# Three reorderings of small steps in a fused attention and expert kernel: first second-weight split, open groups, low parts at the border

## The chip, the cores and the metric

The kernel runs on one core of a Trainium2 chip. The metric is the device time of one execution in microseconds, as the median of several runs. The engines are TensorE (PE; its weight loads are PEld), VectorE (DVE), ScalarE (ACT), GpSimd (POOL) and SyncE (SP), which here issues all DMAs.

## What is computed

All inputs and outputs are float32. With 2 batches of 576 tokens, 8 heads of 64, a model width of 512:

```python
# 1. attention: pooled (means over 4 tokens) plus local (|i - j| < 4), per head
x = repeat(softmax(q_d @ k_d.T / 8) @ v_d, 4) + softmax(where(|i-j|<4, q @ k.T / 8, -1e9)) @ v
# 2. first network, 512 -> 2048 -> 512
h = x @ w_in
y = where(h > 0, h, exp(min(h, 0)) - 1) @ w_out
# 3. four experts, 512 -> 1024 -> 512, all on all 1152 tokens, weighted by normalised probabilities
p = domain_probs / (domain_probs.sum(-1) + 1e-9)
out = sum(p[:, e] * (relu(y @ w1[e]) @ w2[e]) for e in range(4))
```

## The kernel before, in words

**High and low parts.** Each float32 matrix product is done as three matmuls on rounded values (fp32r): high by high, high by low, low by high. So each operand is split. ScalarE copies the raw tile to a rounded high part (`wa_hi`, `wb_hi`, `x_hi`, `h_hi`), and GpSimd (weights, and layer 3's inputs) or VectorE (`x_lo`, `h_lo`) subtracts it from the raw tile for the low part. The helper `product` issues the three matmuls of each chunk (lines 437 to 439), `product2` the same for the experts (514 to 518). A weight tile is 128 x 4 x 512: four chunks of 128 x 512, for which `wa_` holds a block of the first weights of a network and `wb_` one of the second weights. There is one raw, one high and one low buffer of each. SyncE loads the next block into `wa_raw` or `wb_raw` when all four low parts of the block before are done (`next_wa`, `next_wb`, lines 286 and 291).

**Stages.** (1) Attention of the first batch, four head pairs one after the other, with nothing else on TensorE. (2) The first network for batch 0, as four blocks of 512 hidden units; each has 16 groups of 12 matmuls of 288 columns. Groups 0 to 7 make hidden tiles (and wait for `wa_lo`), groups 8 to 15 apply the second weights (and wait for `wb_lo`). Attention of one head pair of the second batch is spread between the groups (`mixed_block1`). The first of the four blocks is written out by itself, the others are a loop. (3) The same network for batch 1, again four blocks, the first by itself. (4) The experts: eight halves (expert and half of its hidden units). Each half has two steps, `step2(j, b)`, for the two sets of tokens, and then `down2`, which multiplies the hidden tiles by the second weights, four token tiles first and five later, each 12 matmuls of 512 columns. `step2` needs sums of weight quarters beside the weights: GpSimd makes these with four additions and subtractions (`add_w2`, lines 1201 to 1206), in `wa_raw` and a small area, and ScalarE and GpSimd split them together with the weights (`split_w2`, `split_wa2`).

**Order.** Each engine runs its own list, written out by hand, and waits on semaphores that count what others finished. Nothing is reordered at run time.

**Group and PSUM banks in layer 2.** Groups go through four PSUM banks. Group g of the first eight is followed by ScalarE's relu and exp (`elu_parts`, lines 710 and 713), VectorE's maximum (941), ScalarE's `h_hi` (719) and VectorE's `h_lo` (947), and only then is the bank free: group g + 4 waits for `h_lo` of group g (`bank_free1`). ScalarE's list for group g is: `elu_parts(g)`, then what stands in `between` for that group (parts of attention), then `elu_hi(g - 1)`, then for g = 0, 1, 2 one, one and two of the four `wb_hi` copies (`split_wb`, line 702).

**Open groups (`up_first`).** In the first block of either batch the last input tile `x` (chunk 3) comes late. So TensorE takes the first `OPEN` = 4 groups side by side: the matmuls of chunks 0, 1 and 2 for all four groups, then those of chunk 3 for all four. Between chunk 2 and chunk 3 of batch 0 stand the input transposes of the next head pair (line 355).

**Before the first mixed block** ScalarE ends stage 1 with `split_x(3, 0, 3)`, the last input tile, and then waits for the transposes (`copy_qT`).

**The border from layer 2 to 3.** `step2(0, 0)` and `step2(0, 1)` run, then `down2` of half 0, four tiles, then `step2(1, 0)`. GpSimd's list there is: `split_y(1)` (low parts of the second batch's inputs), `add_w2(1)`, `split_wb(8)` (the four `wb_lo` of half 0's second weights), `split_wa2(1)`. The last three are the first pass of a loop over the halves. ScalarE makes the four `wb_hi` of half 0 in `step2(0, 1)`, the last of them after two `h_hi`, and then splits the next half's weights and sums (`next_weights2`). VectorE copies the gate column of the expert (`gate_now`, line 1022) before the first use in `down2` (line 1026).

Of the kernel before, what the change touches and what calls it, by code (L numbers as in the profile page):

```python
# [45 lines left out]
FC = FB // 128  # L46
BLOCKS1 = D_FF // FB
# [4 lines left out]
GROUPS1 = T1 * FC + T1 * KC  # L52
# [9 lines left out]
HALVES = EXPERTS * HALVES2  # L62
# [13 lines left out]
DOWN2_BANKS = (7, 6)  # L76
BANK_A, BANK_B, BANK_C = (0, 3), (1, 4), (2, 5)
OUT_SPLIT = QT * SPANS[1][1]
OPEN = 4

# [13 lines left out]
def program(nc, q, k, v, w_in, w_out, probs, w1, w2, out):  # L96
# [12 lines left out]
    with ExitStack() as ctx:  # L109
# [3 lines left out]
        def sem(name):  # L113
            return ctx.enter_context(nc.semaphore(name))
# [98 lines left out]
        s_raw_ready, s_hi_ready, s_lo_ready = sem("s_raw_ready"), sem("s_hi_ready"), sem("s_lo_ready")  # L213
# [124 lines left out]
        def _(pe):  # L338
# [5 lines left out]
            def turn_in(u, mode):  # L344

                if mode == MIXED:
                    pe.wait_ge(out_free, 2 * u + OUT_CREDIT)
                for n, src in enumerate((q_in[held(u)], k_in[held(u)])):
                    pe.wait_ge((q_loaded, k_loaded)[n][held(u)], 32 * loads(u))
                    if n == 1 and mode == ALONE and u >= 2:  # L350

                        pe.wait_ge(attnT_p_copied, 2 * (u - 1))
                        pe.wait_ge(attnT_copied, 3 * (u - 1) - 1)
                    for c in range(NLT):
                        last = nc.tensor.transpose(psum[:, IN_BANKS[mode][n] + c // 3, LT * (c % 3):LT * (c % 3 + 1)],  # L355
                                                   src[:, c, :], ident[0:LT, 0:LT])
                    last.then_inc(in_turned, 1)
# [116 lines left out]
            def up_first(w, b):  # L474

                for k in range(KC):
                    pe.wait_ge(wa_lo_ready, KC * w + k + 1)
                    if b == 0 and k == KC - 1:
                        turn_in(HALF_PAIRS, MIXED)
                    pe.wait_ge(x_lo_ready, KC * b + k + 1)  # L480
                    for g in range(OPEN):
                        if k == 0:
                            bank_free1(w, g)
                        cols, t = slice(128 * g, 128 * (g + 1)), slice(b * SEQ, b * SEQ + N1)
                        bank = psum[:, MOE_BANKS[g], 0:N1]
                        nc.tensor.matmul(bank, wa_hi[:, k, cols], x_hi[:, k, t], start=(k == 0), stop=False)
                        nc.tensor.matmul(bank, wa_hi[:, k, cols], x_lo[:, k, t], start=False, stop=False)
                        last = nc.tensor.matmul(bank, wa_lo[:, k, cols], x_hi[:, k, t], start=False, stop=(k == KC - 1))
                        if k == KC - 1:
                            last.then_inc(group_done, 1)  # L490

            def mixed_block1(i, u):

                if isinstance(i, int):
                    up_first(i, 0)
                for g in range(GROUPS1):
                    if not isinstance(i, int) or g >= OPEN:
                        group1(i, 0, g)
                    if g == 0 and not isinstance(i, int):
                        turn_in(u, MIXED)  # L500
                    elif g == 3:
                        score(u, 0, MIXED)
                        score(u, 1, MIXED)
                    elif g == 5:
                        score(u, 2, MIXED)
                    elif g in (7, 9, 11):
                        turn_attn(u, (g - 7) // 2, MIXED)
                    elif g == 13:
                        mix(u, MIXED)
# [128 lines left out]
                mixed_block1(i, i + HALF_PAIRS)  # L638

            up_first(BLOCKS1, 1)  # L640
            for g in range(OPEN, GROUPS1):
                group1(BLOCKS1, 1, g)
            with pe.Fori(BLOCKS1 + 1, 2 * BLOCKS1) as w:
                for g in range(GROUPS1):
# [9 lines left out]
        def _(act):  # L654
            def copy_qT(u, mode):
                first = IN_BANKS[mode][0]
                act.wait_ge(in_turned, 2 * u + 1)

                nc.scalar.activation(qT[:].rearrange("p (a n) -> p a n", a=2), psum[:, first:first + 2, 0:HALF], ACT.Copy,
                                     scale=HD ** -0.5).then_inc(qT_copied, 1)  # L660
# [29 lines left out]
            def split_x(u, b, i):  # L690
                act.wait_ge(out_free, OUT_CREDIT + 2 * u + 2)
                nc.scalar.copy(x_hi[:, i, b * SEQ:(b + 1) * SEQ], x_sum[:]).then_inc(x_hi_ready, 1)
# [23 lines left out]
            def elu_hi(w, b, g):  # L716
                t0 = b * SEQ + N1 * (g // FC)
                act.wait_ge(elu_ready, UP1 * w + g + 1)
                nc.scalar.copy(h_hi[:, g % FC, t0:t0 + N1], psum[:, MOE_BANKS[g % 4], 0:N1]).then_inc(h_hi_ready, 1)

            def group1(w, b, g, between=(), next_wa=True):
                if g < UP1:
                    elu_parts(w, g)
                for step, *where in between:
                    step(*where)
                if 1 <= g <= UP1:
                    elu_hi(w, b, g - 1)
                if g < FC - 1:
                    split_wb(w, g)
                if g == FC - 2:  # L730
                    split_wb(w, FC - 1)
                if next_wa and g >= UP1 and g < UP1 + KC:
                    split_wa(w + 1, g - UP1, groups_before1(w) + UP1)
# [98 lines left out]
            for u in range(HALF_PAIRS):  # L832
                for j in range(3):
                    if j > 0:
                        copy_attnT(u, j, ALONE)
                    if u + 1 < HALF_PAIRS:
                        exponentiate(u + 1, j, ALONE)
                if u + 2 < HALF_PAIRS:
                    copy_qT(u + 2, ALONE)
                copy_pooled(u, ALONE)  # L840
                if u == 0:
                    first_wa(0)
                if u + 1 < HALF_PAIRS:
                    first_wa(u + 1)
                split_x(u, 0, u)
            copy_qT(HALF_PAIRS, MIXED)

            def mixed_block1(i, u):

                between = {  # L850
                    0: [] if isinstance(i, int) else [(copy_qT, u, MIXED)],
                    3: [(exponentiate, u, 0, MIXED)],
                    4: [(exponentiate, u, 1, MIXED)],
                    6: [(exponentiate, u, 2, MIXED)],
                    10: [(copy_attnT, u, 1, MIXED)],
                    12: [(copy_attnT, u, 2, MIXED)],
                    14: [(copy_pooled, u, MIXED)],
                    15: [(split_x, u, 1, i)],
                }
                for g in range(GROUPS1):  # L860
                    group1(i, 0, g, between.get(g, ()))

            mixed_block1(0, HALF_PAIRS)
            with act.Fori(1, BLOCKS1) as i:
# [269 lines left out]
        def _(pool):  # L1134
# [31 lines left out]
            def split_wb(w):  # L1166
                for c in range(FC):
                    split_w(w, c, wb_raw, wb_hi, wb_lo, wb_hi_ready, wb_lo_ready)
# [29 lines left out]
            def add_w2(j):  # L1198

                pool.wait_ge(wa_loaded, 16 * (2 * BLOCKS1 + j + 1))  # L1200
                nc.gpsimd.tensor_tensor(s_raw[:, S1], wa_quad(1, 0), wa_quad(1, 1), ALU.add).then_inc(s_raw_ready, 1)
                pool.wait_ge(s_raw_ready, 4 * j + 1)
                nc.gpsimd.tensor_tensor(s_raw[:, S2], s_raw[:, S1], wa_quad(0, 0), ALU.subtract).then_inc(s_raw_ready, 1)
                nc.gpsimd.tensor_tensor(wa_quad(1, 0), wa_quad(0, 0), wa_quad(1, 0), ALU.subtract).then_inc(s_raw_ready, 1)
                pool.wait_ge(s_raw_ready, 4 * j + 3)
                nc.gpsimd.tensor_tensor(s_raw[:, S4], wa_quad(0, 1), s_raw[:, S2], ALU.subtract).then_inc(s_raw_ready, 1)
# [6 lines left out]
            def split_wa2(j):  # L1213

                w = 2 * BLOCKS1 + j
                split_w(w, 0, wa_raw, wa_hi, wa_lo, wa_hi_ready, wa_lo_ready)
                split_w(w, 1, wa_raw, wa_hi, wa_lo, wa_hi_ready, wa_lo_ready)
                split_s(j, S2)
                split_w(w, 2, wa_raw, wa_hi, wa_lo, wa_hi_ready, wa_lo_ready)
                split_w(w, 3, wa_raw, wa_hi, wa_lo, wa_hi_ready, wa_lo_ready)  # L1220
                split_s(j, S1)
                split_s(j, S4)
# [54 lines left out]
            add_w2(0)  # L1277
            split_wa2(0)
            split_y(1)
            with pool.Fori(0, HALVES - 1) as j:  # L1280
                pool.wait_ge(s_lo_ready, 3 * j + 3)
                add_w2(j + 1)
                split_wb(j + 2 * BLOCKS1)
                split_wa2(j + 1)
# [22 lines left out]
```

## Time and profile before

| | us |
|---|---|
| median of 3 runs | 676.61 (676.55 to 676.63) |
| the profiled execution | 676.82 |
| its span, first to last instruction | 674.8 |
| TensorE busy in it | 655.0 (97%) |
| mean granted TensorE clock | 0.994 of full speed |

The profile is one execution of the program, taken by the hardware profiler. All times in it count from the start of the span; the execution takes 2.0 us beside the span. L12 is line 12 of the kernel. A row of the timeline reads: start, duration, engine, line, operation, output and inputs, shape, count and, in brackets, how long the engine sat idle before it and what ended that. A granted clock of 1.00 is 2.4 GHz, of 0.50 is 1.2 GHz.

### The profile page before, as it was taken

How to read it: one execution, taken by the hardware profiler on the slowest of the kernel's cores; microseconds unless marked ns; L12 is line 12 of the kernel's file. 1: busy time of each engine (PE TensorE's matmuls, PEld its weight loads, DVE VectorE, ACT ScalarE, POOL GpSimd, SP SyncE). 2: the span in 40 equal slices, each digit the busy share in tenths (PEclk: the TensorE clock that was granted, in tenths of full speed). 3: DMA queues.
4: the chain of work that ended last, by engine and by line, in shares of the span. 5: the costliest groups of instructions: out<-in, count | busy, mean ns of one | idle time of the engine just before them, and what ended most of it. 6: DMA issues, size and time to landing. Idle time of an engine off the chain costs nothing.

```text
span 674.8 us, 12939 instructions
## 1 busy us (share of the span) xinstructions
PE 655.0 (97%) x4750; PEld 601.8 (89%) x4756; DVE 325.1 (48%) x714; ACT 277.6 (41%) x759; POOL 304.4 (45%) x266
## 2 busy tenths in 40 slices
PE   7988999999989999998999999999999999999998
PEld 4767999999989999997889989998998899899886
DVE  4784454545444433465345436534544454365342
ACT  3756565656555653745115214214133152152110
POOL 3584343535349832879605606325337147061110
PEclk9999999999989999999999999999999999999999
DMA  9944070605102123110201201103003012010012
GB/s 173 240 80 157 5 196 6 192 3 159 62 28 99 63 72 115 63 63 34 92 1 63 64 0 62 62 0 124 0 0 124 0 49 75 1 62 1 1 48 93
DMA packets 51488, 46.11 MB, mean 68 GB/s; under 512 B 31616, under 2 KB 33920, under 8 KB 51456
## 3 DMA queue, kind: packets, MB, share of 16 engines
q1 hardware_dynamic: 51456, 45.67, 23.0%
q8 instruction: 21, 0.34, 0.2%
q14 instruction: 11, 0.09, 0.0%
HBM read 43.30 MB, written 2.36 MB: 68 GB/s over the span
## 4 chain that ended last, share of the span: by engine, by line
PE 85%; ACT 6%; DVE 4%; POOL 3%; issue 1%; DMA 1%; SPq 0%; POOLq 0%; ACTq 0%; DVEq 0%
PE psum L437 19%; PE psum L439 18%; PE psum L438 18%; PE psum L516 8%; PE psum L518 8%; PE psum L514 8%; ACT attn L670 2%; ACT attn_p L670 1%; DVE neg_max L899 1%; POOL x_lo L1190 1%; PE psum L429 1%; PE psum L355 1%; PE psum L408 1%; POOL wb_lo L1160 1%; PE psum L374 1%
## 5 line engine op out<-in xcount | busy, mean ns | idle before, releaser
L1160 POOL TENSOR_TENSOR wb_lo<-wb_raw,wb_hi 128x512 fp32r<-128x512 f32 x64 | 82.0, 1294 | 215.3 <-ACT wb_hi L702 215.3
L1026 DVE SCALAR_TENSOR_TENSOR o_acc<-psum,gate_now,o_acc 128x512 f32<-128x512 f32 x72 | 54.1, 751 | 129.8 <-PE psum L439 129.4
L437 PE MATMUL psum<-wb_hi,h_hi 128*128 128x512 f32 x288 | 112.9, 392 | 2.6 <-POOL wb_lo L1160 2.6
L439 PE MATMUL psum<-wb_hi,h_lo 128*128 128x512 f32 x288 | 112.9, 392 | 0.0
L438 PE MATMUL psum<-wb_lo,h_hi 128*128 128x512 f32 x288 | 112.8, 392 | 0.0
L759 ACT ACTIVATE h_hi<-psum 128x320 fp32r<-128x320 f32 (+1 forms) x128 | 52.4, 411 | 87.8 <-DVE psum L998 40.4
L1160 POOL TENSOR_TENSOR wa_lo<-wa_raw,wa_hi 128x512 fp32r<-128x512 f32 x60 | 76.0, 1295 | 23.6 <-ACT wa_hi L746 14.1
L765 ACT COPY sums<-psum 128x256 f32<-128x256 f32 (+1 forms) x32 | 12.8, 399 | 163.3 <-PE psum L518 163.3
L437 PE MATMUL psum<-h_hi,wb_hi 128*128 128x288 f32 x256 | 76.8, 300 | 0.0
L439 PE MATMUL psum<-h_hi,wb_lo 128*128 128x288 f32 x256 | 75.4, 294 | 0.0
L438 PE MATMUL psum<-h_lo,wb_hi 128*128 128x288 f32 x256 | 75.4, 294 | 0.0
L437 PE MATMUL psum<-x_hi,wa_hi 128*128 128x288 f32 x224 | 68.3, 305 | 4.9 <-DVE h_lo L947 4.5
L437 PEld LDWEIGHTS psum<-wb_hi,h_hi 128*128 128x128 f32 x288 | 54.4, 189 | 13.9 <-issue 2.9
L438 PE MATMUL psum<-x_lo,wa_hi 128*128 128x288 f32 x224 | 66.7, 298 | 0.0
L439 PE MATMUL psum<-x_hi,wa_lo 128*128 128x288 f32 x224 | 66.7, 298 | 0.0
L439 PEld LDWEIGHTS psum<-wb_hi,h_lo 128*128 128x128 f32 x288 | 54.4, 189 | 11.4
L438 PEld LDWEIGHTS psum<-wb_lo,h_hi 128*128 128x128 f32 x288 | 54.5, 189 | 11.1
L980 DVE SCALAR_TENSOR_TENSOR h_lo<-psum,h_hi 128x320 fp32r<-128x320 f32 (+1 forms) x128 | 54.9, 450 | 17.0 <-ACT h_hi L759 17.0
L518 PE MATMUL psum<-x_hi,wa_lo 128*128 128x256 f32 (+1 forms) x192 | 56.8, 296 | 0.0
L516 PE MATMUL psum<-x_lo,wa_hi 128*128 128x256 f32 (+1 forms) x192 | 56.7, 295 | 0.0
L514 PE MATMUL psum<-x_hi,wa_hi 128*128 128x256 f32 (+1 forms) x192 | 56.6, 295 | 0.0
L941 DVE SCALAR_TENSOR_TENSOR psum<-sums,psum 128x288 f32<-128x288 f32 x64 | 29.6, 462 | 48.0 <-ACT sums L713 47.8
(146 smaller groups left out, 1548.3 us busy)
## 6 DMA issues: line engine op xcount, KB each, us to landing
wa_raw<-in_moe_w_in SPq DMA_DIRECT2D x8, 1024.0 KB, 5.5
wb_raw<-in_moe_w_out SPq DMA_DIRECT2D x8, 1024.0 KB, 5.0
wa_raw<-in_moe_w SPq DMA_DIRECT2D x8, 1024.0 KB, 4.9
wb_raw<-in_moe_w SPq DMA_DIRECT2D x8, 1024.0 KB, 5.0
out<-o_acc SPq DMA_DIRECT2D x9, 256.0 KB, 2.0
q_in<-in_q SPq DMA_DIRECT2D x10, 144.0 KB, 3.5
k_in<-in_k SPq DMA_DIRECT2D x10, 144.0 KB, 4.0
v_in<-in_v SPq DMA_DIRECT2D x5, 288.0 KB
```

Source lines behind the costliest of these rows:

```text
L437: nc.tensor.matmul(bank_cols, w_hi(n), x_hi_(n), start=(n == 0), stop=False)
L438: nc.tensor.matmul(bank_cols, w_hi(n), x_lo_(n), start=False, stop=False)
L439: last = nc.tensor.matmul(bank_cols, w_lo(n), x_hi_(n), start=False, stop=(n == chunks - 1))
L514: nc.tensor.matmul(bank, w_op[0][:, k, :], x_op[0][:, k, :], start=(start and k == 0), stop=False, skip_group_check=True)
L516: nc.tensor.matmul(bank, w_op[0][:, k, :], x_op[1][:, k, :], start=False, stop=False, skip_group_check=True)
L518: last = nc.tensor.matmul(bank, w_op[1][:, k, :], x_op[0][:, k, :], start=False, stop=(stop and k == 1), skip_group_check=True)
L670: last = nc.scalar.activation(out[:, c, :], psum[:, bank, width * (c - c0):width * (c - c0 + 1)], ACT.Exp, bias=neg_max[:, stat:stat + 1], ...
L759: nc.scalar.activation(h_hi[:, 2 * fh + p, t0 + width * th:t0 + width * (th + 1)], psum[:, bank[p], 0:width], ACT.Relu).then_inc(h_hi_read ...
L941: nc.vector.scalar_tensor_tensor(bank, elu_exp[:, g % 2, 0:N1], -1.0, bank, ALU.add, ALU.max).then_inc(elu_ready, 1)
L980: nc.vector.scalar_tensor_tensor(h_lo[at], bank(banks, p), 0.0, h_hi[at].bitcast(F32), ALU.max, ALU.subtract).then_inc(h_lo_ready, 1)
L1026: nc.vector.scalar_tensor_tensor(o_acc[:, m, :], psum[:, DOWN2_BANKS[(MT * half + m) % 2], :], gate_now[:, m:m + 1], o_acc[:, m, :], ALU.m ...
L1160: nc.gpsimd.tensor_tensor(lo[:, c, :], raw[:, c, :], hi[:, c, :].bitcast(F32), ALU.subtract).then_inc(lo_ready, 1)
```

## The change

It has three parts. (A) ScalarE makes the four `wb_hi` of the first block between the last `split_x` of stage 1 and `copy_qT`, and no longer in groups 0 to 2 of the first mixed block; the loop blocks keep theirs. (B) `up_first` takes two groups side by side for the second batch, where it took four; groups 2 and 3 then run as ordinary groups. Batch 0 keeps four. (C) GpSimd's first pass of the loop over the halves is written out, with `split_wb(8)` ahead of `add_w2(1)`; the other passes keep their order.

```diff
-OPEN = 4
+OPEN = (4, 2)
...
-                    for g in range(OPEN):
+                    for g in range(OPEN[b]):
                         if k == 0:
                             bank_free1(w, g)
...
-                    if not isinstance(i, int) or g >= OPEN:
+                    if not isinstance(i, int) or g >= OPEN[0]:
                         group1(i, 0, g)
...
             up_first(BLOCKS1, 1)
-            for g in range(OPEN, GROUPS1):
+            for g in range(OPEN[1], GROUPS1):
                 group1(BLOCKS1, 1, g)
...
-            def group1(w, b, g, between=(), next_wa=True):
+            def group1(w, b, g, between=(), next_wa=True, this_wb=True):
...
-                if g < FC - 1:
+                if this_wb and g < FC - 1:
                     split_wb(w, g)
-                if g == FC - 2:
+                if this_wb and g == FC - 2:
                     split_wb(w, FC - 1)
...
                 split_x(u, 0, u)
+            for c in range(FC):
+                split_wb(0, c)
             copy_qT(HALF_PAIRS, MIXED)
...
-                    group1(i, 0, g, between.get(g, ()))
+                    group1(i, 0, g, between.get(g, ()), this_wb=not isinstance(i, int))
...
             split_y(1)
-            with pool.Fori(0, HALVES - 1) as j:
+            split_wb(2 * BLOCKS1)
+            pool.wait_ge(s_lo_ready, 3)
+            add_w2(1)
+            split_wa2(1)
+            with pool.Fori(1, HALVES - 1) as j:
                 pool.wait_ge(s_lo_ready, 3 * j + 3)
                 add_w2(j + 1)
                 split_wb(j + 2 * BLOCKS1)
```

## Rows read from the trace of the kernel before

**Rows 1.** The page's first part: busy us (share of span) and instructions of each engine.

```profile
PE 655.0 (97%) x4750; PEld 601.8 (89%) x4756; DVE 325.1 (48%) x714; ACT 277.6 (41%) x759; POOL 304.4 (45%) x266
```

**Rows 2.** The waits of TensorE: line waited for, us in total, times, longest.

```profile
PE psum L437 <- DVE h_lo L947: 4.5, 3, 1.9
PE psum L437 <- POOL wb_lo L1160: 2.6, 1, 2.6
```

**Rows 3.** Windows: stretch, length, busy (count) of PE, PEld, DVE, ACT, POOL; PEclk, DMA.

```profile
195.90:199.30 3.40, 3.40 (x16) 3.40 (x15) 1.74 (x5) 3.33 (x10) 3.09 (x3) 0.50 0.03 7
...
314.80:317.40 2.60, 0.00 (x0) 0.01 (x1) 2.39 (x6) 2.16 (x6) 2.60 (x3) 1.00 0.00 0
318.80:322.20 3.40, 3.40 (x10) 2.65 (x9) 0.40 (x1) 0.62 (x2) 3.40 (x4) 0.51 0.80 292
322.20:325.60 3.40, 3.40 (x16) 2.77 (x16) 1.10 (x2) 0.00 (x0) 3.40 (x3) 1.00 0.24 30
```

**Rows 4.** Timeline of TensorE, first mixed block: start, us, line, tiles, idle before.

```profile
64.89 0.40 PE L437 MATMUL psum<-x_hi,wa_hi 128*128 128x288 f32 x1 [1.18 <-DVE h_lo L947]
...
68.18 0.40 PE L437 MATMUL psum<-x_hi,wa_hi 128*128 128x288 f32 x1 [1.43 <-DVE h_lo L947]
```

**Rows 5.** Timeline of ScalarE, first mixed block.

```profile
54.58 0.65 ACT L659 ACTIVATE qT<-psum 128x576 f32<-128x576 f32 x1 [3.52 <-PE psum L355]
...
59.57 1.14 ACT L702 CAST wb_hi<-wb_raw 128x512 fp32r<-128x512 f32 x2
```

**Rows 6.** Timeline of VectorE, first mixed block.

```profile
57.20 0.98 DVE L941 SCALAR_TENSOR_TENSOR psum<-sums,psum 128x288 f32<-128x288 f32 x2
...
64.38 0.46 DVE L947 TENSOR_TENSOR h_lo<-psum,h_hi 128x288 fp32r<-128x288 f32 x1 [1.55 <-ACT h_hi L719]
...
67.67 0.46 DVE L947 TENSOR_TENSOR h_lo<-psum,h_hi 128x288 fp32r<-128x288 f32 x1 [1.39 <-ACT h_hi L719]
```

**Rows 7.** All that touches wb_raw in the first 60 us.

```profile
L302 SPq DMA_DIRECT2D wb_raw<-in_moe_w_out x1: 578/578/578, 29.0 to 29.0; - x1
...
DMA to landing us min/median/max: 6.3/6.3/6.3
```

**Rows 8.** Timeline of TensorE, second batch's first block: first matmul, restart after the wait.

```profile
186.88 0.29 PE L486 MATMUL psum<-x_hi,wa_hi 128*128 128x288 f32 x1
...
195.30 0.40 PE L437 MATMUL psum<-x_hi,wa_hi 128*128 128x288 f32 x1 [1.95 <-DVE h_lo L947]
```

**Rows 9.** Timeline of ScalarE, same stretch.

```profile
192.21 0.41 ACT L710 ACTIVATE sums<-psum 128x288 f32<-128x288 f32 x1 [4.74 <-PE psum L488]
```

**Rows 10.** Timeline of VectorE, same stretch.

```profile
187.64 0.76 DVE L934 TENSOR_TENSOR x_lo<-x_sum,x_hi 128x576 f32 x1
...
198.50 0.45 DVE L947 TENSOR_TENSOR h_lo<-psum,h_hi 128x288 fp32r<-128x288 f32 x1
```

**Rows 11.** Timeline of GpSimd at the border.

```profile
305.39 1.56 POOL L1195 TENSOR_TENSOR t_lo<-h_spare,t_hi 128x640 fp32r<-128x640 f32 x1
...
312.15 5.02 POOL L1160 TENSOR_TENSOR wb_lo<-wb_raw,wb_hi 128x512 fp32r<-128x512 f32 x4
...
323.32 2.57 POOL L1210 TENSOR_TENSOR s_lo<-y_acc,s_hi 128x512 fp32r<-128x512 f32 x2
```

**Rows 12.** Timeline of ScalarE at the border.

```profile
312.18 0.61 ACT L702 CAST wb_hi<-wb_raw 128x512 fp32r<-128x512 f32 x1
...
330.96 0.37 ACT L765 COPY sums<-psum 128x256 f32<-128x256 f32 x1 [11.54 <-PE psum L518]
```

**Rows 13.** Two small VectorE operations, all in the span: ns min/median/max, first and last start.

```profile
L909 DVE TENSOR_SCALAR sums<-sums x24: 140/161/3577, 12.0 to 173.2; 128x3 f32<-128x3 f32 x8, 128x4 f32<-128x4 f32 x8, 128x5 f32<-128x5 f32 x8
...
L1022 DVE COPY gate_now<-gate x8: 160/462/1275, 316.4 to 622.5; 128x4 f32 x3, 128x5 f32 x3, 128x4 f32<-128x4 f32 x1, 128x5 f32<-128x5 f32 x1
```

**Rows 14.** Timeline of VectorE at the longest of L909.

```profile
40.50 3.58 DVE L909 TENSOR_SCALAR sums<-sums 128x4 f32<-128x4 f32 x1
```

**Rows 15.** Timeline of GpSimd in the same stretch.

```profile
40.68 2.50 POOL L1245 TENSOR_TENSOR wa_lo<-wa_raw,wa_hi 128x512 fp32r<-128x512 f32 x2
```

## The prediction, written before the changed kernel was run

> **What bounds the kernel now.** The busy shares come first: TensorE is busy for 655.0 of 674.8 us [rows 1], no other engine for half of that. So time is to be had only where TensorE waits, or where its clock is low. Next the waits of TensorE [rows 2]. Two lines in them touch this change: 4.5 us in three waits for `h_lo` (L947), and one wait of 2.6 us for `wb_lo` (L1160). The timeline places the three: two in the first mixed block, 1.18 and 1.43 us [rows 4], and one of 1.95 us in the second batch's first block [rows 8]. The 2.6 us lie at the border, 314.8 to 317.4 [rows 3]. Then the granted clock: it is 0.50 (the lower level, 1.2 GHz) from 195.9 to 199.3 and again from 318.8 to 322.2 [rows 3]. What TensorE did before both: it had just come back from the two longest of these waits. After the waits of 1.18 and 1.43 us it stays at full speed.
>
> A stretch of 3.4 us at a clock of 0.50 does 1.7 us of full-speed work, so it costs up to 1.7. By counts, 10 matmuls of 512 columns fit in where 16 fit in the 3.4 us behind it [rows 3]: 6 of 0.21 us each, so 1.3 (matmuls that reach over an edge count on both sides, which makes this low). I take 1.5 for each stretch.
>
> **Part A, ScalarE in the first mixed block.** The four `wb_hi` copies go from between `elu_parts` and `elu_hi` to an idle stretch. One takes 0.61 alone [rows 12] and two take 1.14 [rows 5], so each further one adds 0.52 or so to the queue and the four 2.08. The cover at the new place: ScalarE idles 3.52 us, until the transposes end at 54.5 [rows 5]. 2.08 fits, with 1.4 to spare. The data is there: the load was issued at 29.0 and landed 6.3 later [rows 7], and ScalarE gets there at about 51.1. Moving it costs nothing in the sum; were the load late, `copy_qT` and all behind it would slip by as much.
>
> What is gained is not 2.08. The first `h_hi` waits for VectorE, whose first maximum starts at 57.20 behind its reductions of the new head pair [rows 6]; that doesn't move, so the copy ahead of `h_hi` 0 (0.52) was hidden. The other three are on the chain: ScalarE's exps, VectorE's maxima, the attention exps that wait for a row maximum behind them, then `h_hi` 2 and `h_lo` 2. That chain comes 1.56 earlier. `h_lo` 2 then ends at 64.38 + 0.46 - 1.56 = 63.28, and TensorE wants it at 64.89 - 1.18 = 63.71 [rows 4, 6]: that wait is gone. `h_lo` 3 ends at 67.67 + 0.46 - 1.56 = 66.57 and releases group 7 at 66.6 in place of 68.18. That wait stays, at about 1.4 - 0.4 = 1.0 to 1.3 us. From there TensorE has no wait for `h_lo` in this block, so what counts is how much earlier group 7 starts: **1.56**. Bounds: 0, if something else on ScalarE or VectorE takes the place of the copies, and 2.08, all four. GpSimd's four `wb_lo` go along, to about 51.7 to 57; `wb_lo` is wanted only from group 8 on. VectorE's last `x_lo` starts as they begin; TensorE needs it only for chunk 3.
>
> **Part B, two open groups.** No instruction is added or removed on TensorE; 36 matmuls of chunks 0 to 2 ahead of chunk 3 become 18, and group 0 ends sooner. Spacing: 48 matmuls from 186.88 until the wait begins at 193.35 (195.30 - 1.95) [rows 8], 0.132 us each with the tail of the last taken off. Chunk 3 is then wanted at 186.88 + 18 x 0.132 = 189.25. The last `x_lo` ends at 187.64 + 0.76 = 188.40 [rows 10], so 0.85 is left; no wait. Group 0 ended with its 39th matmul and now ends with the 21st: 18 x 0.132 = 2.37 earlier. ScalarE's relu of group 0, which waited 4.74 us for it at 192.21 [rows 9], starts at 189.84, and its list and VectorE's replies follow with the same spacing, since groups 1 to 3 are ready when asked for (group 3 at 193.4, asked for at 194.8). `h_lo` 0 ends at 192.9; TensorE wants it at 193.2, and goes on. `h_lo` 1 ends about 0.3 ahead of need. `h_lo` 2 ends at 198.50 + 0.45 - 2.37 = 196.58 [rows 10], and TensorE, with 12 matmuls of 0.133 to a group, wants it at 193.2 + 2 x 1.6 = 196.4. So a new wait of 0.2 to 0.3. Then `h_lo` 3 (197.7) is ahead of need (198.2). Gain: the wait of 1.95, the half-clock stretch that followed it, 1.5, and 0.1 for the slow first matmul of a restart (0.40 against 0.29, rows 8), less 0.3: **3.25**. Bounds: 0 (the ELU chain is as late as before), and 1.95 + 1.7 + 0.1 = 3.75.
>
> **Part C, the border.** Now: GpSimd ends `split_y` at 306.95, does the four weight sums until 312.15 (5.20), then the four `wb_lo` until 317.17 [rows 11], and `down2` starts at 317.40. Then: three `wb_lo` of 1.26 run from 306.95 to 310.8. The fourth waits for ScalarE's last `wb_hi`, which ends at 312.18 + 0.61 = 312.79 [rows 12]. It ends at about 314.15, and with the 0.23 from its end to the first matmul seen now, `down2` can start at 314.4. TensorE is through with `step2(0, 1)` at 314.8 [rows 3]. The wait is gone, by a margin of some 0.3. Gain 2.6, the clock stretch 1.5, the restart 0.1: **4.2**. Bounds: 2.6 - 0.5 = 2.1 if the fourth low part is late and the clock still falls, and 4.4.
>
> What is moved back: the sums now run from 314.15 to 319.35, and the seven low parts behind them (317.17 to 325.89 now, 8.72) from 319.35 to 328.1. ScalarE, which splits the next weights right behind `step2(0, 1)`, waits for the third sum until about 318. Behind it stands only the copy for `step2(1, 0)`, which comes at 330.96 now [rows 12] and some 4.2 earlier then. SyncE's next load of `wa_raw` waits for the last `wa_lo` which ends at 323.4 now (rows 11), and so slips to about 325.7; the sums that read it are wanted a whole half later. `step2(1, 0)` itself starts at about 325.7. It wants the first two `wa_lo` at once (there at 321.9), the first sum 1.4 later (323.2 against 327.1), the other `wa_lo` at 328.5 (325.7), the second sum at 330.0 (326.9) and the third at some 332.8 (328.1). The smallest margin is 2.8, so this costs nothing. If it didn't hold, TensorE would wait by the difference.
>
> **Sum.** 1.56 + 3.25 + 4.2 = 9.0 of the profiled execution's 676.82, so 667.8. The median of the runs is 0.2 below that execution, so the forecast is 667.6.
>
> **Rival 1, the clock stays low once.** The clock falls after TensorE was idle for a while, and with A a wait of about 1.2 us stays, with B one of 0.3. If one of them, or another place, still has a half-clock stretch, 1.5 is not gained: 669.1. For it: the dip follows idle time, and some is left. Against it: two waits of 1.18 and 1.43 us close together had none.
>
> **Rival 2, B gives nothing.** If VectorE or ScalarE is slower with groups 2 and 3 in their ordinary place, each of groups 4 to 7 waits for its `h_lo`. With 3.25 gone the time is 670.9. Against it: the spacing of ScalarE's list is its own, not TensorE's.
>
> **Rival 3, slower: VectorE's gate copy is shut out by GpSimd.** A small VectorE operation on SBUF, L909, has a median of 0.16 [rows 13], and once took 3.58, from 40.50 to 44.08 [rows 14], while GpSimd ran two `wa_lo` and went on [rows 15]. The gate copy takes from 0.16 to 1.27, the first of them at 316.4 [rows 13]. With the change GpSimd is busy without a pause from 312.9 to 328.1. Should the copy from 316.4 get in only at the end, the first `down2` result is taken out of PSUM at 328.3 + 0.75 = 329.1. TensorE has two banks for these and stops after two tiles, at 314.7 + 2 x 2.73 = 320.2: a wait of 8.9, with a half-clock stretch of 1.5 behind it. That turns C from 4.2 gained to 6.2 lost, the sum to -1.4 and the time to 678.0. It costs something from the point at which the copy gets in later than 319.3. Against it: no gate copy took over 1.27 [rows 13], which is one GpSimd operation (1.26), and at 316.4 GpSimd had 9 us of work without a pause before it in this run too [rows 11]. So the next end of an operation, at 316.8 or 318.1, is likely, and it costs nothing.
>
> On this the Trainium skill, page "SBUF — State Buffer", section "SBUF: two separate sides", says that the port pair which VectorE (in some forms of operation) shares with GpSimd is an exclusive lock for a whole instruction, and that the loser blocks fully. The 3.58 and the 1.27 agree with the blocking. The page does not say who gets in next, on which the rival hangs; by one instruction per lock the copy loses at most 1.3 us and the sum stays.
>
> **Rival 4, a part doesn't act,** for instance A, if the third and later steps of its chain hang on something else: 669.2 without A.
>
> **How the numbers follow.** Forecast 0.70. Rival 1 0.10, rival 2 0.06, rival 4 (with C's smaller forms) 0.09, rival 3 0.03, no change that can be told 0.02. About 0.2%, or 1.35 us, is what a measurement of this kernel can tell from no change. The range: below, all upper ends for the clock (0.2 each) and the restart terms give 667.0, and I allow 0.4 more for waits that I count as remaining; above, it takes in rivals 1 and 4: 666.6 to 669.4. Faster 0.95, same 0.02, slower 0.03.
>
> **What would show it.** In the changed kernel's waits, no wait for `wb_lo` on TensorE, and the three for `h_lo` down to one of about 1.2 us near 66 and a short one near 195. Granted clock 1.00 throughout but for the ends. The first `wb_hi` at about 51. `down2` starting within 0.2 us of the end of `step2(0, 1)`. I am wrong if a wait for the next weights (`wa_lo`, `s_lo`) or for a free `down2` bank turns up behind the border, or if a clock of 0.50 remains.

## The result, and the profile after

| | before | changed |
|---|---|---|
| median of 4 runs, us | 676.62 (676.55 to 676.85) | 667.39 (667.23 to 668.98) |
| profiled execution | 676.82 | 667.47 |
| its span | 674.8 | 665.4 |
| TensorE busy in it | 655.0 | 651.9 |

The ratio is 0.9868, with a 95% interval of 0.9851 to 0.9885. The forecast was 667.6, with a range of 666.6 to 669.4.

The page of the changed kernel, its first part and the clock strip (40 slices, each digit in tenths of full speed). Against [rows 1] TensorE is busy for 3.1 us less on the same 4750 matmuls; that is about what the two half-clock stretches cost. No slice of the clock strip is below 9 (90% or more of full speed).

```profile
PE 651.9 (98%) x4750; PEld 599.6 (90%) x4756; DVE 324.4 (49%) x714; ACT 277.7 (42%) x759; POOL 304.5 (46%) x266
...
PEclk9999999999999999999999999999999999999999
```

The waits of TensorE. The line for `wb_lo` of [rows 2] is gone, and 4.5 us in three waits for `h_lo` are down to one of 1.0. The first line was there before too, with the same 2.6.

```profile
PE psum L370 <- DVE qTs L894: 2.6, 4, 1.3
...
PE psum L437 <- DVE h_lo L949: 1.0, 1, 1.0
```

First mixed block: ScalarE (start, duration, line, tiles, idle before). The four copies stand in what was idle for 3.52 us [rows 5]; 1.43 of it is left.

```profile
51.12 2.18 ACT L702 CAST wb_hi<-wb_raw 128x512 fp32r<-128x512 f32 x4
54.73 0.66 ACT L659 ACTIVATE qT<-psum 128x576 f32<-128x576 f32 x1 [1.43 <-PE psum L355]
```

VectorE, the first maximum and `h_lo` 2 and 3. The maximum has not moved against [rows 6] but for the offset of this run (57.35 for 57.20); the two `h_lo` are 1.52 and 1.53 earlier.

```profile
57.35 0.82 DVE L943 SCALAR_TENSOR_TENSOR psum<-sums,psum 128x288 f32<-128x288 f32 x2
...
62.86 0.46 DVE L949 TENSOR_TENSOR h_lo<-psum,h_hi 128x288 fp32r<-128x288 f32 x1 [1.56 <-ACT h_hi L719]
...
66.14 0.46 DVE L949 TENSOR_TENSOR h_lo<-psum,h_hi 128x288 fp32r<-128x288 f32 x1 [1.39 <-ACT h_hi L719]
```

TensorE. Only the wait before group 7 is left, and group 7 starts 1.52 us earlier than in [rows 4].

```profile
66.66 0.40 PE L437 MATMUL psum<-x_hi,wa_hi 128*128 128x288 f32 x1 [0.99 <-DVE h_lo L949]
```

The second batch's first block: ScalarE's relu of group 0. It waited 4.74 us in [rows 9].

```profile
188.32 0.41 ACT L710 ACTIVATE sums<-psum 128x288 f32<-128x288 f32 x1 [2.37 <-PE psum L488]
```

VectorE: the last `x_lo`, `h_lo` 0 and `h_lo` 2.

```profile
186.13 0.76 DVE L936 TENSOR_TENSOR x_lo<-x_sum,x_hi 128x576 f32 x1
...
190.91 0.45 DVE L949 TENSOR_TENSOR h_lo<-psum,h_hi 128x288 fp32r<-128x288 f32 x1
...
194.62 0.45 DVE L949 TENSOR_TENSOR h_lo<-psum,h_hi 128x288 fp32r<-128x288 f32 x1
```

TensorE: the first matmul, the last of group 5 and the first of group 6. The wait of [rows 8] is gone. Between the last two rows lies 0.38 where the spacing is 0.13: the new wait of 0.25 for `h_lo` 2, which ends at 195.07. It is so short that the matmul before it still drains, and no view lists it as idle.

```profile
185.36 0.29 PE L486 MATMUL psum<-x_hi,wa_hi 128*128 128x288 f32 x1
...
194.75 0.29 PE L439 MATMUL psum<-x_hi,wa_lo 128*128 128x288 f32 x1
195.13 0.40 PE L437 MATMUL psum<-x_hi,wa_hi 128*128 128x288 f32 x1
```

The border: GpSimd. Three `wb_lo`, a pause of 2.13 for ScalarE's last `wb_hi`, the fourth, then the sums, and the last low parts of the next weights until 323.28.

```profile
302.04 3.81 POOL L1162 TENSOR_TENSOR wb_lo<-wb_raw,wb_hi 128x512 fp32r<-128x512 f32 x3
307.98 1.30 POOL L1162 TENSOR_TENSOR wb_lo<-wb_raw,wb_hi 128x512 fp32r<-128x512 f32 x1 [2.13 <-ACT wb_hi L702]
309.23 1.30 POOL L1203 TENSOR_TENSOR y_acc<-wa_raw 128x512 f32<-128x512 f32 x1
...
314.48 2.55 POOL L1162 TENSOR_TENSOR wa_lo<-wa_raw,wa_hi 128x512 fp32r<-128x512 f32 x2
...
320.73 2.55 POOL L1212 TENSOR_TENSOR s_lo<-y_acc,s_hi 128x512 fp32r<-128x512 f32 x2
```

TensorE: `down2` follows `step2(0, 1)` without a gap.

```profile
309.59 0.31 PE L518 MATMUL psum<-t_hi,wa_lo 128*128 128x320 f32 x1
309.74 0.39 PE L437 MATMUL psum<-wb_hi,h_hi 128*128 128x512 f32 x1
```

ScalarE: the last `wb_hi`; the next weights, held up for 2.27 us by the third sum; and the first copy of `step2(1, 0)`.

```profile
307.29 0.61 ACT L702 CAST wb_hi<-wb_raw 128x512 fp32r<-128x512 f32 x1
...
313.18 1.14 ACT L746 CAST wa_hi<-wa_raw 128x512 fp32r<-128x512 f32 x2 [2.27 <-POOL wa_raw L1206]
...
321.58 0.37 ACT L765 COPY sums<-psum 128x256 f32<-128x256 f32 x1 [4.65 <-PE psum L518]
```

VectorE: the gate copy, and the first `down2` result.

```profile
311.54 0.39 DVE L1024 COPY gate_now<-gate 128x4 f32 x1
312.70 0.75 DVE L1028 SCALAR_TENSOR_TENSOR o_acc<-psum,gate_now,o_acc 128x512 f32<-128x512 f32 x1 [0.77 <-PE psum L439]
```

Read as milestones (before, after, gained so far, in us): group 7 of the first mixed block 68.18, 66.66, 1.52; first matmul of the second batch 186.88, 185.36, 1.52; group 8 of that block 203.32, 198.44, 4.88; first `step2` matmul 292.36, 287.48, 4.88; first `down2` matmul 317.40, 309.74, 7.66; first copy of `step2(1, 0)` 330.96, 321.58, 9.38; end of the span 9.4. Between these points nothing is won or lost.

### The profile page after: what moved, and what is told of

The parts are those of the page before. It is cut to its first block, busy times and chain, and to the rows that moved or that the text cites. A ratio compares the mean times of both kernels' runs of the same rounds, so it can differ in the third digit from the quotient of the medians.

```text
span 665.4 us, 12923 instructions
## 1 busy us (share of the span) xinstructions
PE 651.9 (98%) x4750; PEld 599.6 (90%) x4756; DVE 324.4 (49%) x714; ACT 277.7 (42%) x759; POOL 304.5 (46%) x266
## 3 DMA queue, kind: packets, MB, share of 16 engines
HBM read 43.30 MB, written 2.36 MB: 69 GB/s over the span
## 4 chain that ended last, share of the span: by engine, by line
PE 88%; ACT 5%; DVE 5%; issue 1%; POOL 0%; ACTq 0%; DVEq 0%
PE psum L437 19%; PE psum L439 18%; PE psum L438 18%; PE psum L516 9%; PE psum L518 9%; PE psum L514 9%; ACT attn L670 2%; ACT attn_p L670 1%; DVE neg_max L901 1%; PE psum L355 1%; PE psum L342 1%; PE psum L429 1%; PE psum L408 1%; PE psum L374 1%; DVE sums L911 1%
## 5 line engine op out<-in xcount | busy, mean ns | idle before, releaser
L759 ACT ACTIVATE h_hi<-psum 128x320 fp32r<-128x320 f32 (+1 forms) x128 | 52.4, 411 | 87.8 <-DVE psum L1000 40.4
L437 PE MATMUL psum<-x_hi,wa_hi 128*128 128x288 f32 x232 | 69.9, 301 | 1.4 <-DVE h_lo L949 1.0
L438 PE MATMUL psum<-x_lo,wa_hi 128*128 128x288 f32 x232 | 68.3, 294 | 0.0
L439 PE MATMUL psum<-x_hi,wa_lo 128*128 128x288 f32 x232 | 68.3, 294 | 0.0
```

The lines of the kernel that those rows point to most:

```text
L437: nc.tensor.matmul(bank_cols, w_hi(n), x_hi_(n), start=(n == 0), stop=False)
L438: nc.tensor.matmul(bank_cols, w_hi(n), x_lo_(n), start=False, stop=False)
L439: last = nc.tensor.matmul(bank_cols, w_lo(n), x_hi_(n), start=False, stop=(n == chunks - 1))
L759: nc.scalar.activation(h_hi[:, 2 * fh + p, t0 + width * th:t0 + width * (th + 1)], psum[:, bank[p], 0:width], ACT.Relu).then_inc(h_hi_read ...
```

## Experiments

**The clock in the runs.** The timed runs carry a mean granted clock, and it takes few values. Over the 38 runs of the kernel before that were made beside the experiments:

| mean clock | runs | median us | from, to |
|---|---|---|---|
| 1.000 | 4 | 674.29 | 674.14, 674.44 |
| 0.997 | 12 | 675.33 | 675.03, 676.14 |
| 0.994 or 0.995 | 18 | 676.99 | 676.56, 678.54 |
| 0.992 | 4 | 678.69 | 678.61, 678.99 |

The profiled execution with its two half-clock stretches in the kernel's body has 0.994. I read the levels as no, one, two and three such stretches; a step is 1.0 to 1.7 us. The twelve kept profiles bear this out as far as two: the one with two stretches in the body has 0.994, the three with one (a_alone, c_alone, open_4_1) have 0.997, and the eight with none have 0.999 or 1.000. Three stretches were seen in no profile. Comparing kernels at the same level takes most of the clock out; not all of it, since a stretch does not cost the same everywhere (1.0 near 193, 1.64 at the border, as shown further on), and since some runs lie 1 us and more above the others of their level (676.14, 678.41, 678.54 here). "At full clock" below means runs at 0.999 or 1.000; the last stretch of half clock in many profiles begins only when TensorE has ended and costs nothing.

**a_alone.** ScalarE's part only, with the copies in groups 0 to 2 of that block left out:

```diff
+            for c in range(FC):
+                split_wb(0, c)
             copy_qT(HALF_PAIRS, MIXED)
```

> Part A alone (ScalarE's four wb_hi of the first block moved ahead of copy_qT). Theory: only the three copies behind the first h_hi were on the chain, so group 7 of the first mixed block starts about 1.5 us earlier and the time is 675.1, with both stretches at half clock (near 194 and 317) still there. Rival (all four copies count): 674.5. Rival (the gain is given back at the next waits, near 193 or at the border): 676.6.

Median 674.76 of 12 runs, ratio 0.9975 (0.9959 to 0.9990). None was at full clock. At 0.997 the median is 674.13, 1.2 under the kernel before at that level; at 0.995 it is 675.44, 1.55 under. That fits 1.5 and not 2.1. The wait near 193 and the one at the border are there as before. Two of the eight runs at 0.997 lie higher, at 675.27 and 675.75. The spread from 1.2 to 1.55 is no wider than the difference between two places of a stretch. The profile (0.997) has one half-clock stretch where two were expected. TensorE's restart near 193, and then windows behind both waits (length; busy us and count of PE, PEld, DVE, ACT, POOL; granted clock; DMA share and GB/s):

```profile
193.61 0.40 PE L437 MATMUL psum<-x_hi,wa_hi 128*128 128x288 f32 x1 [1.94 <-DVE h_lo L949]
```

```profile
193.80:197.20 3.40, 3.28 (x24) 3.05 (x23) 1.58 (x4) 3.30 (x10) 3.10 (x3) 1.00 0.03 7
316.20:319.60 3.40, 3.40 (x9) 2.65 (x8) 0.60 (x1) 0.54 (x2) 3.40 (x4) 0.50 0.73 273
```

The same wait of 1.94 us is followed by full clock here, where [rows 3] had 0.50. And there is a second wait in this block that the kernel before did not show, 0.24 us listed before group 6. The rows from the first matmul to group 8:

```profile
185.19 0.29 PE L486 MATMUL psum<-x_hi,wa_hi 128*128 128x288 f32 x1
...
196.79 0.29 PE L439 MATMUL psum<-x_hi,wa_lo 128*128 128x288 f32 x1
197.32 0.40 PE L437 MATMUL psum<-x_hi,wa_hi 128*128 128x288 f32 x1 [0.24 <-DVE h_lo L949]
...
200.63 0.29 PE L437 MATMUL psum<-h_hi,wb_hi 128*128 128x288 f32 x1
```

This is the same code for the block as in the kernel before, at full clock: 15.44 us from first matmul to group 8, against 16.44 (186.88 to 203.32) with the half-clock stretch. So the stretch cost 1.0 there. It slowed some 14 matmuls from a spacing of 0.13 to 0.24, about 1.5 in all, but the slower TensorE then reached group 6 at 200.12, when `h_lo` 2 had been ready since 198.95 [rows 10], and the stop before group 6 (0.40 over the spacing of 0.13, and 0.11 for the slower second matmul) did not occur.

**b_alone.** `OPEN = (4, 2)` only.

> Part B alone (two open groups in the second batch's first block). Theory: the wait of 1.95 us near 193 goes and takes the half-clock stretch behind it along: 3.3 us less, 673.3, with one half-clock stretch left at the border. Rival (only the wait goes, the clock falls anyway): 674.7.

Median 672.06 of 6 (17 runs of the kernel before beside it: 676.91), ratio 0.9932 (0.9916 to 0.9948): more than expected. Five of the six runs were at full clock, median 672.03, which is 2.26 under 674.29; the sixth, at 0.997, has 673.09. So the part gives 2.3 at equal clock; the rest of the 4.9 between the medians is clock. TensorE at the border, and the window behind:

```profile
313.99 0.49 PE L437 MATMUL psum<-wb_hi,h_hi 128*128 128x512 f32 x1 [2.62 <-POOL wb_lo L1160]
```

```profile
315.40:318.80 3.40, 3.40 (x17) 2.81 (x16) 0.75 (x1) 0.61 (x2) 3.40 (x4) 1.00 0.91 301
```

The wait of 2.62 us is untouched, and no half-clock stretch follows. This prices the stretch at the border too: from the first `down2` matmul to the first of `step2(1, 0)` it is 11.01 here (313.99 to 325.00) and was 12.65 before (317.40 to 330.05), so 1.64. The theory that such a wait brings one, and its removal 1.5 us, is too simple.

**c_alone.** `split_wb(8)` ahead of the sums, only.

> Part C alone (w2 low parts ahead of the next weight sums at the border). Theory: the wait of 2.6 us goes and the half-clock stretch behind it too: 4.2 us less, 672.4, with one half-clock stretch left near 196. Rival (only the wait goes): 673.9. Rival (the sums come too late for step2(1, 0)): a wait of TensorE for wa_lo or s_lo behind the border.

Median 672.48 of 6, ratio 0.9936 (0.9919 to 0.9954). One run at full clock: 671.40, 2.9 under 674.29; four at 0.997, median 672.49, 2.8 under their level; one at 0.995, 674.18, also 2.8 under. The expected 672.4 was met. TensorE waits for no `wa_lo` or `s_lo` behind the border. The profile has the stretch near 196:

```profile
196.50:199.90 3.40, 3.40 (x17) 3.40 (x16) 1.86 (x6) 3.20 (x9) 3.10 (x4) 0.50 0.03 7
```

**after_again.** The changed kernel, 6 more runs.

> The changed kernel once more, unchanged. Theory: 667.3 in most runs, the three parts add up (1.5 + 3.3 + 4.2 = 9.0 off 676.6). One of four runs so far was at 668.98 with a mean clock of 0.997 where the others had 0.999 to 1.000. If a half-clock stretch now and then comes behind one of the waits that are left, some of these runs are again 1.5 us above the rest at a lower mean clock; if that was chance, all lie within 0.3 us.

Median 667.44 (667.25 to 670.79), ratio 0.9870 (0.9849 to 0.9891). With the 4 first runs: 8 of 10 at full clock, median 667.38; two at 0.997, at 668.98 and 670.79. The parts at equal clock give 1.2 to 1.55, 2.3 and 2.9, in sum 6.4 to 6.75; together they give 674.29 - 667.38 = 6.9. The run at 670.79 is 3.4 above the others with the mean clock of one stretch, which one stretch does not explain.

**sums_3_first.** A wait of known size put back at the border:

```diff
-            split_wb(2 * BLOCKS1)
-            pool.wait_ge(s_lo_ready, 3)
-            add_w2(1)
+            # wb_lo 0, 1, 2, then sums 1 to 3, then wb_lo 3, then sum 4
```

> The changed kernel, but at the border three of the four weight sums run ahead of the last wb_lo. A wait of known size put back: wb_lo 3 ends near 311.1 in place of 309.3, and TensorE waits some 1.5 us for it. Theory (the clock falls only behind some waits, and whether it does differs from run to run): runs at clock 1.000 lie near 668.9, runs with a half-clock stretch there some 1.3 to 1.7 above. Rival 1 (a wait of 1.5 us never brings a half-clock stretch): all near 668.9. Rival 2 (always): all near 670.4.

Median 668.98 of 6 (668.67 to 672.34). Five at full clock, 668.97; one at 0.997, 672.34. The wait came to 1.29 us, on the same line as the 2.6 before:

```profile
311.17 0.49 PE L437 MATMUL psum<-wb_hi,h_hi 128*128 128x512 f32 x1 [1.29 <-POOL wb_lo L1162]
```

It costs 1.6 in time at full clock (668.97 against 667.38), which shows that this is the wait that part C removes. Rival 2 is out, since five of six have no stretch. Between the theory and rival 1 this does not decide: of the sixth run only the mean clock is known, not where its stretch lay, and it is 3.4 above the others where the theory had 1.3 to 1.7.

**open_4_3, open_4_1.** `OPEN = (4, 3)` and `(4, 1)`.

> The changed kernel with three open groups in the second batch's first block in place of two. Theory: group 0 ends 9 matmuls (1.19 us) later, the whole chain of ScalarE and VectorE with it; h_lo 0, about 0.3 us early in the changed kernel, comes 0.8 to 0.9 late and h_lo 2 about 1.1 late: TensorE waits some 1.1 us in all, 668.5 in runs at clock 1.000, with no half-clock stretch in the profile. Rival (the wait is all or nothing, as with four): 669.4 and a wait of 1.95.

> The changed kernel with one open group in the second batch's first block. Theory: nine matmuls of chunks 0 to 2 take 1.2 us, chunk 3 is wanted some 0.3 us before the last x_lo is there, and the chain behind group 0 had no wait left to lose: 667.6 to 667.7 in runs at clock 1.000, with a wait of 0.3 on x_lo. Rival (the earlier group 0 still gains): under 667.2.

With three: 668.71 of 6, five at full clock with 668.70, which is 1.3 above the changed kernel; the sixth, at 0.997, has 670.15. The listed waits of TensorE in that block come to 1.0 in all, before groups 4 and 6:

```profile
192.44 0.40 PE L437 MATMUL psum<-x_hi,wa_hi 128*128 128x288 f32 x1 [0.76 <-DVE h_lo L949]
...
196.15 0.40 PE L437 MATMUL psum<-x_hi,wa_hi 128*128 128x288 f32 x1 [0.24 <-DVE h_lo L949]
```

With one: 668.33 of 6; the three at full clock have 667.59, 0.2 above the changed kernel. The wait for `x_lo` is there with 0.32:

```profile
188.30 0.37 PE L486 MATMUL psum<-x_hi,wa_hi 128*128 128x288 f32 x1 [0.32 <-DVE x_lo L936]
```

The other three runs are at 0.997 (668.88 to 669.46), and the profile is one of them. Its half-clock stretch is not at the edit at all, but in the first attention stage, in which TensorE waits often; just before the clock fell, from 10.60 to 13.98, it was busy for 2.11 us. The profiles of the kernel before and of the changed one have the same 2.11 us between these times, but full clock behind. The profile of open_4_1:

```profile
10.60:13.98 3.38, 2.11 (x42) 1.59 (x41) 1.65 (x6) 2.41 (x14) 0.78 (x1) 1.00 1.16 206
13.98:17.39 3.41, 3.41 (x17) 2.30 (x17) 2.19 (x6) 2.17 (x11) 0.79 (x2) 0.50 1.03 210
```

**hi_first.** In group 4 of the first mixed block ScalarE does `elu_hi(3)` ahead of the attention exps.

> The changed kernel, and in group 4 of the first mixed block ScalarE makes h_hi of group 3 ahead of the attention exps, not behind them. Theory: what is left of the wait before group 7 (0.99 us at 66) is h_hi 3 standing behind exps that themselves wait for a row maximum; h_lo 3 then ends near 65.2, TensorE wants it at 65.7, the wait goes and 666.4 is seen in runs at clock 1.000. Rival (the exps, now later, delay the attention that TensorE turns next): 667.4 or more, with a wait on L396 or L408.

Median 667.07 of 5; three at full clock, 666.93, which is 0.45 under the changed kernel, half of what was expected. The other two, at 0.997, have 668.83 and 669.70. No new wait on L396 or L408 is listed behind the edit, so the rival is out. The wait before group 7 is gone, but one of 0.38 for `h_lo` 4 has come before group 8. VectorE makes `h_lo` 4 behind the maximum of group 5, and group 5's relu on ScalarE still stands behind the exps' wait for the row maximum (0.60 here, 0.89 in the changed kernel), so this part of the chain came forward by only 0.3:

```profile
68.02 0.37 PE L437 MATMUL psum<-h_hi,wb_hi 128*128 128x288 f32 x1 [0.38 <-DVE h_lo L952]
```

**open_2_2, hi_first_open_2_2.** `OPEN = (2, 2)`, without and with that edit.

> The changed kernel with two open groups in the first batch too. Theory: what held for the second batch holds here: group 0 ends sooner, ScalarE's and VectorE's chains come about 2 us earlier, the 0.7 us wait for qTs and most of the 0.99 us wait for h_lo go: 666.0 in runs at clock 1.000. Rival (the transposes and copy_qT are the chain, since the last x_lo ends only at 52.2 and ScalarE has its four copies until 53.3): a wait before chunk 3, and 667.4 or more.

> Both of these. Theory: no wait for h_lo or qTs is left in the first mixed block: 665.7 in runs at clock 1.000, faster than either kernel of the case. Rival: the two take away the same wait, so this is no better than the better of the two.

With two open groups in both batches: 665.32 of 5, four at full clock, median 665.29 (666.0 was expected), 2.1 under the changed kernel at full clock and ratio 0.9857 (0.9833 to 0.9881) to the kernel before. TensorE's transposes move ahead from 54.0 to 51.6, and the row of the first scores is no longer behind a wait; from 49 to 70 us TensorE is busy all the time (19.3 of these 21 us in the changed kernel):

```profile
51.61 0.66 PE L355 MATMUL psum<-ident,q_in 96*128 96x96 f32 x6
...
56.72 0.95 PE L374 MATMUL psum<-kTs,qTs 64*64 64x144 f32 x12
```

```profile
49.00:70.00 21.00, 21.00 (x196) 19.98 (x192) 13.18 (x33) 17.11 (x57) 9.89 (x11) 1.00 0.46 130
```

With the ScalarE edit on top it is 665.30 of 5, and at full clock (three runs) 665.14 against 665.29; the other two, at 0.997, have 666.74 and 667.48. The rival holds within 0.15: they take away the same wait.

## Why the prediction was right, and where not

**Part A, 1.56: held.** The chain came 1.52 earlier, the first of four copies was hidden behind VectorE's maximum, the wait before group 6 went and that before group 7 stayed at 1.0. a_alone gives 1.2 to 1.55 at equal clock; its mean clock does not say where a run's stretch lay, so it cannot be read closer.

**Part B, 3.25: 3.36 in the profile, but made up otherwise.** The forecast was 1.75 by waits and restarts and 1.5 by the clock; it is 2.36 and 1.00. a_alone gives the split: at full clock and with four open groups the block takes 15.44 to group 8, with two 13.08 (185.36 to 198.44). Two things were missing in the 1.75. The wait of 1.95 is counted from where the matmul before it is drained; from start to start TensorE lost 2.10 (2.23 between two matmuls where the spacing is 0.13), so 0.16 more. And at full clock the four open groups also cost the stop before group 6, 0.51 with its restart, which the trace of the kernel before could not show, because its slow clock covered it. The new wait with its restart costs 0.36 where 0.3 was put. In sum 1.75 + 0.16 + 0.51 - 0.06 = 2.36. The detail held: the new short wait for `h_lo` 2 was forecast at 0.2 to 0.3 and is 0.25. The 0.85 us of cover for the last `x_lo` is borne out by open_4_1, which takes away nine matmuls (1.2) of it and gets a wait of 0.32. Rival 2, that B gives nothing because each of groups 4 to 7 waits for its `h_lo`, is out: the 0.25 before group 6 is the only such wait, and the chain behind group 0 does follow its start. open_4_3 ends group 0 nine matmuls (1.19) later, the way from the first matmul to group 8 grows by 1.19, from 13.08 to 14.27, and the time at full clock by 1.3.

**Part C, 4.2: 4.50 in the profile**, 2.78 up to the first `down2` matmul and 1.72 behind it. b_alone, with the wait and at full clock, splits it: 2.87 by the wait and the restart, where the forecast had 2.7, and 1.64 by the clock. The fourth `wb_lo` ended at 309.28 and TensorE was through at 309.74. The work moved back cost nothing: `step2(1, 0)` starts near 320.7, the first `wa_lo` are there at 317.03, the last low part at 323.28.

**Rival 3, the gate copy shut out, is out.** It took 0.39 beside a GpSimd that ran through from 307.98 to 323.28. The long one was no accident of that trace: in all twelve profiles the same small operation, at 40.4 to 41.9, takes 3.56 to 3.58, and it ends with the third GpSimd operation behind its start. It was seen at that place alone, and what lets VectorE in after one operation at the border and only after several there stays open.

**The step that was mis-sized is the clock.** The prediction added 1.5 for each half-clock stretch as if each came with its wait. The profile of before has two. By their mean clock 18 of the 38 runs of that kernel have two, 4 have three, and 16 have none or one; b_alone kept its wait of 2.62 with five of six runs at full clock. And the two together cost 2.64 in the profile (1.00 and 1.64), not 3.0. At full clock the change is worth 6.9, not the 6.0 that the waits and restarts of the forecast make (1.56 + 1.75 + 2.7), and the clock 2.3 of the median's 9.2, not 3.0. The profiles say the same: 1.52 + 2.36 + 2.87 = 6.75 by waits and 2.64 by the clock make the 9.4 of the span. The waits were put 0.7 to 0.9 too low, most of it in part B, and the clock 0.4 to 0.7 too high. That the sum of 9.0 came out within 0.2 of the median's 9.2 is thus in part luck. Which waits go, in which order and where, was foreseen.

**Rival 1 happened, in 2 of 10 runs.** A half-clock stretch still turns up now and then. open_4_1's profile shows one place for it, in the attention stage ahead of all three edits, where the kernel before has the same waits. Whether the runs at 668.98 and 670.79 had theirs there isn't known, as both traces of the changed kernel are of runs at full clock. What decides whether a wait is followed by half clock is open too. That runs of the same code have it in some executions and not in others is shown by the mean clocks of the 38 runs, and that a wait of 1.94 or 2.62 can pass without it by the profiles of a_alone and b_alone.

## What to carry to other kernels

A small step in an in-order engine's list costs what it delays behind it. The same four copies cost 1.5 us in one place and nothing 5 us earlier, and which of them count is read from the engine that the next step waits for, not from their sum. Where work is opened side by side to cover a late operand, open only as much as the cover needs, since the rest delays the first result: two groups left 0.85 us of cover to spare in the second batch, and the first batch, left at four, gained another 2.1 us from the same step. When a wait is followed by a stretch of low clock in one profile, price wait and clock apart, and take the clock's part from many runs with their mean clock. A slow stretch can also hide a wait behind it: here the one before group 6, 0.51 with its restart, shows only in the profiles in which the clock stayed up.

## What was not expected of the hardware

The clock differs from run to run of the same code: mean clocks of 1.000, 0.997, 0.994 to 0.995 and 0.992, with times of 674.3, 675.3, 677.0 and 678.7. Waits of about 1.95 and 2.62 us came with a stretch at half clock behind them in some profiles and without in another. A few runs (670.79, 672.34, 668.86 for open_2_2) are 3.4 to 3.6 above their kernel's others at a mean clock of 0.997, more than any single stretch seen has cost (1.0 to 1.64). Other runs at 0.997 are 1.1 to 2.8 above theirs. None of those above 1.64 has a trace, so where their time went is open.
